# A fused three-stage kernel: block 0's convolution sum moved to TensorE, three weight splits moved behind block 0's first steps

## The reference

```python
# 1. softmax over 7 taps, then a causal 7-tap sum per head (x: 2 x 4096 x 192, 8 heads)
w = weight_gen - np.max(weight_gen, axis=-1, keepdims=True)
w = np.exp(w)
w = w / (np.sum(w, axis=-1, keepdims=True) + 1e-09)
out = np.einsum('bshk,bskhg->bshg', w, x_unf)        # x_unf: rows s-6 .. s of x
# 2. first dense stage, 192 -> 2048 -> 192, with a rational activation
h = x @ w_in
P = a[0] + a[1] * h + a[2] * h2 + a[3] * h3
Q = 1.0 + np.abs(b[0]) * np.abs(h) + np.abs(b[1]) * h2
y = (P / (Q + 1e-6)) @ w_out
# 3. second dense stage, 192 -> 1536 -> 192, RMS norm and a gated activation
xn = x / rms * rms_g
g = xn @ w_gate
silu = g * (1.0 / (1.0 + np.exp(-g)))
return (silu * (xn @ w_val)) @ w_out2
```

## Time and profile before

| | us |
|---|---|
| median of 3 runs | 1444.98 |
| profiled execution | 1445.34 |
| its span, first to last instruction | 1443.5 |
| PE busy | 1368.5 (95%) |
| DVE busy | 1247.1 (86%) |
| ACT busy | 1071.0 (74%) |
| POOL busy | 458.4 (32%) |

### The profile page before, as it was taken

The page is one execution under the profiler, slowest core; times in us unless marked ns, Lnnn a source line. Parts: engine busy times, 40 slices in busy tenths (PEclk is TensorE's granted clock), DMA queues, the critical chain, the costliest instruction groups (busy, mean ns, idle before and its releaser), DMA issues.

```text
span 1443.5 us, 20421 instructions
## 1 busy us (share of the span) xinstructions
PE 1368.5 (95%) x7040; PEld 1221.0 (85%) x7040; DVE 1247.1 (86%) x1524; ACT 1071.0 (74%) x1387; POOL 458.4 (32%) x283
## 2 busy tenths in 40 slices
PE   2676999999999999999999999999999999999999
PEld 2465898888898888889898888989888898998988
DVE  6999998989889898988989899898989989888621
ACT  4676877878787787888778788877878787777521
POOL 2935240434324143432414343241434314200000
PEclk9788999999999999999999999999999999999999
DMA  8200001000000100000010000001000000000000
GB/s 232 82 0 31 1 2 41 1 32 11 30 11 0 41 0 30 11 30 11 0 41 0 30 11 30 11 0 41 0 30 11 30 12 0 12 0 1 12 12 11
DMA packets 12514, 32.30 MB, mean 22 GB/s; under 512 B 1604, under 2 KB 7234, under 8 KB 12480
## 3 DMA queue, kind: packets, MB, share of 16 engines
q1 hardware_dynamic: 11744, 31.61, 6.8%
q10 hardware_dynamic: 736, 0.23, 0.1%
HBM read 25.55 MB, written 6.29 MB: 22 GB/s over the span
## 4 chain that ended last, share of the span: by engine, by line
PE 76%; DVE 11%; ACT 7%; issue 4%; DMA 2%; SPq 0%; ACTq 0%; POOL 0%; DVEq 0%; POOLq 0%
PE dn L681 32%; PE bank L672 9%; PE bank L673 8%; PE bank L674 8%; PE bank L675 8%; PE bank L676 8%; DVE den L607 4%; ACT seed L484 2%; PE bank L688 2%; DVE num L599 2%; DVE num L596 1%; DVE num L612 1%; DVE num L618 1%; ACT L484 1%; DMA glu<-in_moe_w_val_dram 1%
## 5 line engine op out<-in xcount | busy, mean ns | idle before, releaser
L681 PE MATMUL dn<-dn_w,num 128*128 128x192 f32 x2048 | 378.8, 329 | 17.1 <-DVE num L618 9.9
L681 PEld LDWEIGHTS dn<-dn_w,num 128*128 128x128 f32 x2048 | 343.5, 192 | 24.3 <-DVE num L618 8.6
L469 ACT ACTIVATE den<-bank,coef 128x512 f32<-128x512 f32 x256 | 175.5, 686 | 175.8 <-PE bank L676 164.6
L681 PE MATMUL dn<-dn_w,glu 128*128 128x192 f32 x1536 | 280.8, 327 | 5.3 <-DVE glu L643 5.3
L681 PEld LDWEIGHTS dn<-dn_w,glu 128*128 128x128 f32 x1536 | 254.3, 190 | 12.9 <-DVE glu L643 8.9
L596 DVE TENSOR_TENSOR num<-num,bank 128x512 f32<-128x512 f32 x256 | 173.9, 679 | 70.1 <-ACT num L471 68.1
L612 DVE SCALAR_TENSOR_TENSOR num<-num,coef,seed 128x1024 f32<-128x1024 f32 x128 | 183.5, 1435 | 40.8 <-ACT seed L490 40.3
L471 ACT ACTIVATE num<-bank,coef 128x512 f32<-128x512 f32 x256 | 199.5, 779 | 0.0
L618 DVE SCALAR_TENSOR_TENSOR num<-den,num 128x1024 f32<-128x1024 f32 x128 | 193.1, 1510 | 0.0
L597 DVE SCALAR_TENSOR_TENSOR den<-den,coef,bank 128x512 f32<-128x512 f32 x256 | 188.9, 738 | 0.0
L599 DVE SCALAR_TENSOR_TENSOR num<-num,coef,bank 128x512 f32<-128x512 f32 x256 | 188.9, 738 | 0.0
(11 more groups left out here) (86 smaller groups left out, 1983.4 us busy)
## 6 DMA issues: line engine op xcount, KB each, us to landing
x_in<-in_x_dram SPq DMA_DIRECT2D x14, 960.0 KB
out_dram<-y_out SPq DMA_DIRECT2D x16, 384.0 KB, 2.3
w_blk<-in_weight_gen_dram SPq DMA_DIRECT2D x14, 112.0 KB, 2.0
dn_w<-in_moe_w_out_dram SPq DMA_DIRECT2D x1, 1536.0 KB, 20.7
dn_w<-in_moe_w_out_dram SPq DMA_DIRECT2D x1, 1152.0 KB, 10.6
num<-in_moe_w_in_dram SPq DMA_DIRECT2D x1, 768.0 KB, 6.6
num<-in_moe_w_in_dram SPq DMA_DIRECT2D x2, 384.0 KB, 8.2
seed<-in_moe_w_gate_dram SPq DMA_DIRECT2D x1, 768.0 KB, 10.0
```

Of the source, the lines that this page charges most:

```text
L681: done = pe.matmul(banks[:, j // 2, j % 2 * D:(j % 2 + 1) * D], acts[:, j * P:(j + 1) * P], w, start=first and j % 2 == 0, stop=last, skip ...
```

## The change

Six things are done.

1. VectorE makes block 0's seven products into separate buffers (`FIRST`) and adds only two pairs of them (products 3 and 4, and 5 and 6): nine instructions in place of fourteen.
2. TensorE flips each of the five remaining tiles with a matmul against the identity and adds them up in PSUM (`flip_and_add`): 12 matmuls a tile (four with 128 output rows into bank 1, eight with 64 into bank 2), 60 in all, in place of eight transposes.
3. Ahead of them TensorE runs 20 products of the identity with itself.
4. ScalarE splits pieces 5, 6 and 7 in iteration 1 of its order, among block 0's `linear`, `abs` and `root` steps.
5. GpSimd keeps only the low half of piece 4 in the opening; those of 5, 6 and 7 follow block 1's convolution.
6. SP's load of block 1's rows and GpSimd's clearing of the halo wait for the seventh product, not for the sum.

```diff
@@ -21,6 +21,7 @@
 EPS_Q = 1.0 + 1e-6
 EPS_RMS = 1e-6
 GLU_RING = 4
+WARM = 20
 
 
 def program(text):
...
@@ -42,9 +43,9 @@
...
-linear 0 1, root 3 2, square 6 2, silu 4 3, linear 1 1, piece 6 0, square 7 2, linear 2 1, linear 3 1,
-piece 7 0, abs 0 1, linear 4 1, silu 5 3, linear 5 1, abs 1 1, root 0 1, square 0 1, square 1 1, linear 6 1,
+silu 6 3, abs 2 1, linear 7 1, piece 5 1, ss 0 2, silu 7 3, abs 3 1, piece 6 1, silu 8 3, root 1 1, piece 7 1, linear 8 1, linear 9 1,
...
@@ -59,7 +60,7 @@
 """)
 
 POOL_PROGRAM = program("""
-add 6 1, less 0 0, norm 0 0, mul 0 0, mul 1 0, mul 2 0, add 1 0, mul 3 0, add 2 0, mul 4 0, rms 0 2, add 3 0,
+add 6 1, piece 5 2, piece 6 2, piece 7 2, less 0 0, norm 0 0, mul 0 0, mul 1 0, mul 2 0, add 1 0, mul 3 0, add 2 0, mul 4 0, rms 0 2, add 3 0,
 mul 5 0, add 4 0, mul 6 0, add 5 0,
 """)
 
...
@@ -287,6 +287,13 @@
         def slots(rows):
             return rows.rearrange("p (j d) -> p j d", j=SLOTS)
 
+
+        FIRST = [slots(prod[:, 0, :]), slots(prod[:, 1, :]), square[:, :, :], y_out[:, :, :], conv_rows,
+                 xn_t[:, :, 0:D], conv_rows]
+
+        def by_slot(rows):
+            return rows.rearrange("p j (h g) -> p j h g", h=H)
+
         def slot_heads(rows):
             return rows.rearrange("p (j h) g -> p j h g", h=H)
 
@@ -340,7 +347,7 @@
                 load_piece(n)
             src, dst = DOWN[0]
             sp.dma_start(dst[:, :, :], src).then_inc(down_in[0], 16)
-            sp.wait_ge(conv0_ready, 1)
+            sp.wait_ge(tap0, K)
             load_first(1)
             sp.dma_start(w_blk[:, :], w_rows[:, 2 * SLOTS * HK:3 * SLOTS * HK]).then_inc(wgen_in, 16)
             src, dst = DOWN[1]
...
@@ -388,11 +395,10 @@
             def normalised_taps(blk, _):
                 normalise(pool, blk)
 
-            pool.wait_ge(conv0_ready, 1)
+            pool.wait_ge(tap0, K)
             pool.memset(x_in[:, 0:(HALO - SLOTS) * D], 0.0).then_inc(halo0, 1)
             pool.wait_ge(wlo0, BY_DVE)
-            for n in range(BY_DVE, len(PIECES)):
-                piece_low(0, n)
+            piece_low(0, BY_DVE)
 
 
             def tap_product(blk, k):
...
@@ -459,7 +466,6 @@
                 piece_high(0, n)
             x_high(0, 0)
             x_high(0, 1)
-            piece_high(0, 5)
             act.wait_ge(coefs, 2)
 
             def linear(blk, c):
@@ -550,22 +556,17 @@
             normalise(dve, 0)
             dve.wait_ge(sm_norm, 1)
 
-            def first_taps(k):
+            def first_product(k):
                 if k == 0:
                     dve.wait_ge(x_in_ready, x_count(0))
-                    dve.tensor_tensor(conv_heads, slot_heads(rows_of(0)), slot_heads(taps_of(0, 0)), ALU.mult).then_inc(tap0, 1)
-                    return
-                if k > 1:
-                    dve.wait_ge(sum0, k - 1)
-                dve.tensor_tensor(by_head(prod[:, 0, :]), rows_of(k), taps_of(k, 0), ALU.mult).then_inc(tap0, 1)
-                dve.wait_ge(tap0, k + 1)
-                product = slots(prod[:, 0, :])
-                if k < K - 1:
-                    dve.tensor_tensor(conv_rows, conv_rows, product, ALU.add).then_inc(sum0, 1)
-                else:
-                    dve.tensor_tensor(conv_twice, conv[:, :, DA:D], product[:, :, DA:D], ALU.add).then_inc(sum0, 1)
-                    dve.wait_ge(sum0, K - 1)
-                    dve.tensor_tensor(conv_rows, conv_rows, product, ALU.add).then_inc(conv0_ready, 1)
+                elif k == 6:
+                    dve.wait_ge(sum0, 1)
+                dve.tensor_tensor(by_slot(FIRST[k]), slot_heads(rows_of(k)), slot_heads(taps_of(k, 0)), ALU.mult)\
+                    .then_inc(tap0, 1)
+
+            def first_sum(k):
+                dve.wait_ge(tap0, k + 2)
+                dve.tensor_tensor(FIRST[k], FIRST[k], FIRST[k + 1], ALU.add).then_inc(sum0, 1)
 
             def x_low(blk, part):
                 wait(dve, xt_hi, blk * 2 + (part + 1))
@@ -575,8 +576,12 @@
                     dve.tensor_tensor(x_b[DB:P, :], bank[XPOSE_BANK[1]][DB:P, :], x_b[DB:P, :], ALU.subtract)\
                        .then_inc(x_ready, 1)
 
-            for k in range(K):
-                first_taps(k)
+            for k in range(5):
+                first_product(k)
+            first_sum(3)
+            for k in range(5, K):
+                first_product(k)
+            first_sum(5)
             for n in range(2):
                 piece_low(n)
             dve.wait_ge(small_in, 16 * 5)
@@ -689,10 +694,7 @@
                 return done
 
             def transposes(blk, part):
-                if isinstance(blk, int) and blk == 0:
-                    pe.wait_ge(conv0_ready, 1)
-                else:
-                    wait(pe, conv_ready, blk)
+                wait(pe, conv_ready, blk)
                 bank_read(blk, "xpose", part)
                 flip(bank[XPOSE_BANK[part]], conv, part).then_inc(xt_ready, 1)
 
@@ -747,9 +749,30 @@
                 wait(pe, glu_ready, blk * 12 + (m + 1))
                 second_layer(dn2, glu[:, m % GLU_RING, :], dn2_w[:, m, :], m == 0, m == N2 - 1).then_inc(dn2_done, 1)
 
+            def flip_and_add(tile, first, last):
+
+                for j in range(SLOTS):
+                    done = pe.matmul(bank[XPOSE_BANK[0]][:, j * P:(j + 1) * P], tile[:, j, 0:DA], ident[:, :],
+                                     start=first and j == 0, stop=last, skip_group_check=True)
+                if last:
+                    done.then_inc(xt_ready, 1)
+                for j in range(SLOTS):
+                    for half in range(0, P, DB):
+                        done = pe.matmul(bank[XPOSE_BANK[1]][half:half + DB, j * P:(j + 1) * P], tile[:, j, DA:D], ident[:, :],
+                                         start=first and j == 0, stop=last, skip_group_check=True)
+                if last:
+                    done.then_inc(xt_ready, 1)
+
             pe.wait_ge(consts, 3)
-            transposes(0, 0)
-            transposes(0, 1)
+            for n in range(WARM):
+                pe.matmul(bank[XPOSE_BANK[0]][:, 0:P], ident[:, :], ident[:, :], start=True, stop=True)
+            for k in (0, 1, 2):
+                pe.wait_ge(tap0, k + 1)
+                flip_and_add(FIRST[k], k == 0, False)
+            pe.wait_ge(sum0, 1)
+            flip_and_add(FIRST[3], False, False)
+            pe.wait_ge(sum0, 2)
+            flip_and_add(FIRST[5], False, True)
             pe.wait_ge(wlo0, 2)
 
             run_iterations(pe, PE_PROGRAM, {
```

More of the change, by code:

```diff
@@ L44 @@
 square 4 2, x_high 1 1, square 5 2, abs 6 2, silu 0 3, silu 1 3, abs 7 2, silu 2 3, silu 3 3, exp 0 0,
-linear 0 1, root 3 2, square 6 2, silu 4 3, linear 1 1, piece 6 0, square 7 2, linear 2 1, linear 3 1,
-piece 7 0, abs 0 1, linear 4 1, silu 5 3, linear 5 1, abs 1 1, root 0 1, square 0 1, square 1 1, linear 6 1,
-silu 6 3, abs 2 1, linear 7 1, ss 0 2, silu 7 3, abs 3 1, silu 8 3, root 1 1, linear 8 1, linear 9 1,
+linear 0 1, root 3 2, square 6 2, silu 4 3, linear 1 1, square 7 2, linear 2 1, linear 3 1,
+abs 0 1, linear 4 1, silu 5 3, linear 5 1, abs 1 1, root 0 1, square 0 1, square 1 1, linear 6 1,
+silu 6 3, abs 2 1, linear 7 1, piece 5 1, ss 0 2, silu 7 3, abs 3 1, piece 6 1, silu 8 3, root 1 1, piece 7 1, linear 8 1, linear 9 1,
 linear 10 1, square 2 1, silu 9 3, abs 4 1, silu 10 3, linear 11 1, silu 11 3, square 3 1, xn_high 0 2,
@@ L215, in build @@
         sum0 = sem("sum0")
-        conv0_ready = sem("conv0_ready")
         tap_ready = sem("tap_ready")
@@ L430, in _ @@
             run_iterations(pool, POOL_PROGRAM, {"mul": tap_product, "add": tap_add, "rms": rms_inverse,
-                                                "less": peak_taken_off, "norm": normalised_taps}, LAST)
+                                                "less": peak_taken_off, "norm": normalised_taps,
+                                                "piece": piece_low}, LAST)
         @block.scalar
```

## The result

The changed kernel takes **1448.74 us** (1447.17 to 1452.04), the kernel before 1444.74 us (1443.11 to 1447.46), medians of 14 runs each. The ratio is 1.0029, with a 95% interval of 1.0022 to 1.0036: 4.0 us slower, and the interval leaves out an equal time. That lies just inside what the prediction calls no change (0.3%), on its slow side, as forecast; forecast were 1447.8 us and +2.8. The profiled execution lasted 1448.36 us (span 1446.6) against 1445.34 (span 1443.5), 3.0 us more.

What follows compares the result with a forecast made beforehand. VectorE was taken to bound the first 150 us, TensorE from 160 us on. An opening gain of 5.3 us against 8.1 us of new waiting gave +2.8 on 1444.98, so 1447.8 us, range 1442.0 to 1451.0.

Steps and rivals of the forecast that it cites:

- The convolution is worth nothing: Opening: 4.3 us off VectorE's convolution turn nearly all into idle time, as `x_high` waits for piece 4; 0.1 us gained.
- TensorE's flips cost nothing: Opening, block 0: 60 flip products are done by 19.5 us, or 24.5 at the lower clock; cost 0, ends 0 and 0.3.
- the rival that gave TensorE too little time: Opening: an fp32 product costs twice a transpose, `horner` 0 at 41.5, about +10.5 us, 1455.5; chance 0.03.
- `horner` 0 at 29.2: Opening, VectorE's first `horner`: starts at about 29.2 us in place of 34.67, 5.5 us earlier.
- Block 1's rows at 39.0: Start of GpSimd's block 1 convolution: its rows land at 39.0 us, with ends of 37.0 and 41.0.
- the main case: Whole kernel: halves block whole, rows land between 38 and 40.5; +1.8 to +4.3 us, 1446.8 to 1449.3; chance 0.52.
- rows at 40.4: Variant of the step-by-step working to the last `py`: block 1's rows landing at 40.4 us give +4.1.
- Three halves block three or four steps, 8.1 us: Behind block 1's convolution, 67 to 83 us: VectorE's `qy`, `newton` and `py` wait for GpSimd's low halves, 8.1 us.
- the rival that a half blocks less than its length: Cheaper collision beside GpSimd's halves, or rows before 38: -1.5 to +1.5 us, 1445.0; chance 0.18.
- the one that it does not collide: GpSimd's halves do not block VectorE: the whole 5.3 us gain stays, 1439.7 us; chance 0.13.
- VectorE has no idle time in which to give it back: After the last `py` near 83 us: the 2.8 us loss stays, and TensorE from 150 us on waits for it.
- in all of every window: Steady part from 160 us: TensorE busy 40.00 of 40.00, a fixed sum that the change does not touch.

Runs made afterwards that it cites:

- e4: The changed kernel's opening alone (flips, identity products, earlier rows), with the splits of pieces 5 to 7 where they were before: 1446.02 us, 1.0005 to the kernel before.
- e6: The changed kernel without the 20 identity products: 1447.33 us, 1.0021 to the kernel before.
- e5: The kernel before with only the splits of pieces 5 to 7 moved on ScalarE and GpSimd: 1448.12 us, 1.0022 to the kernel before.
- e1: The changed kernel with GpSimd clearing the low-half tiles of pieces 5 to 7 instead of subtracting: 1441.98 us, 0.9983 to the kernel before.
- e3: The changed kernel with GpSimd's low-half subtractions cut into 256 columns each: 1442.27 us, 0.9981 to the kernel before.
- e7: The changed kernel with piece 5 split in the opening again on both engines: 1445.35 us, 1.0006 to the kernel before.
- e8: The changed kernel with piece 5 split in the opening and GpSimd's halves cut into 256 columns: 1443.43 us, 0.9987 to the kernel before.
- e10: e9 plus 18 identity products behind the last flip and piece 2's low half ahead of `x_low`: 1431.05 us, 0.9908 to the kernel before.
- e12: e9 with GpSimd's convolution instructions cut in four, one slot each, instead of two: 1432.80 us, 0.9918 to the kernel before.
- e9: e8 with GpSimd's convolution products and additions of blocks 1 to 15 cut in two (one addition excepted): 1431.22 us, 0.9901 to the kernel before.
- e2: The changed kernel with GpSimd's low-half subtractions cut into 512 columns each: 1445.39 us, 0.9998 to the kernel before.
- e11: The kernel before with only GpSimd's convolution instructions of blocks 1 to 15 cut in two: 1434.16 us, 0.9924 to the kernel before.

## Why the prediction came out as it did

The mechanism was right. One term of the sum was mis-sized: when block 1's rows land. It moved the result by about 1.1 us.

- *The convolution is worth nothing.* VectorE was idle 5.94 us behind it, and e4 shows no change. Right.
- *TensorE's flips cost nothing.* Right, but the prices were wrong, and that it did no harm was in part luck. A full fp32 product takes 0.27 us at the higher level for my 0.11. I had misread: the profile has two records for each fp32 product (the 20 identity products show as x40, and the 1024 products of the first stage's `down1` as x2048), so its 24 records of 4.06 us are 12 products of 0.34 us, not 24 of 0.17. Scaled to 128 columns that is 0.23. The premise of the rival that gave TensorE too little time, a product that costs twice a transpose, was thus about true: in e6, at the slower pace, a full one takes 0.49 us for the transposes' 0.24. It did no harm because 40 of the 60 products go into 64 rows and cost half (0.13, or 0.24 at the slower pace), and because all ran at the higher level; even at e6's mixed pace they were done at 23.11. A tile takes 2.1 us instead of 1.4, and the last is still done 3.3 us early. The 20 identity products took 7.00 us for my 4.8 at most and ended 0.85 before the first flip.
- *`horner` 0 at 29.2.* It came at 30.52. Of the 1.3 us, 0.8 is piece 4, whose data landed later in this execution (22.97 for 22.17); it holds `x_high`, and so `up1`, which starts at 26.56 for my 25.8. The other 0.5 is the five matmuls and the `linear` behind them, 2.57 and 1.39 us for my 2.2 and 1.27.
- *Block 1's rows at 39.0.* They came at 40.51, at the edge of the 38 to 40.5 of the main case. **This is the term that was mis-sized**: the prediction's own line for rows at 40.4 reads +4.1, and `horner` 12 came 3.9 us later. GpSimd's convolution took 28.3 us from there, as forecast, ended at 68.77 for my 67.3, and the `py` beside it ended 1.1 after that, so by this working an earlier `horner` 0 alone would have met the same end. (No run has that alone. In e6 `horner` 0 was 1.4 earlier and the rows 0.6, but the convolution took 29.2 us, and `horner` 12 came at 83.31, 0.9 earlier: its length is not as fixed as I took it.) SP's issue of the rows, begun at 17.21, lasted 15.39 us, until 32.60, and the rows were there 7.9 us after that. In e5, which begins at 22.30, it ended at 30.89 and the rows came 7.6 later. In e1, e3, e6, e7, e8, e10 and e12, begun at 16.2 to 17.3, it ended at 32.0 to 32.5 and they came 7.5 to 7.8 later, at 39.7 to 40.2; in e9 it ended at 32.7 and they came at 40.70, in e2 at 35.6 and 43.88. So the landing follows the end of the issue by nearly 8 us, which would have made about my 39.0 of the 31.53 of before; the end is what moved, later by 1.1 us. The prediction had said that the earlier start would not change it. The three runs that start at 22.0 to 22.4 (before, e5, e11) end at 30.8 to 31.5, the eleven that start at 16.2 to 17.3 at 31.6 (e4) to 35.6. That speaks for the earlier start, but the wait was not changed alone, so it stays open.
- *Three halves block three or four steps, 8.1 us.* Measured were 8.0. That each step ends 1.1 us after its half held to 0.1 us. e1 and e3 show by removal that this waiting, and its length, are the loss; e5 that it needs nothing of the convolution; the rival that a half blocks less than its length, and the one that it does not collide, fell. The rule of the Trainium skill (SBUF — State Buffer, Who interferes with whom) is that the shared port pair is an exclusive lock, that whoever comes second is blocked for the whole instruction of the first, and that a VectorE instruction with two SBUF inputs meets it where GpSimd reads SBUF. This trace agrees at 1536 columns: 4.43 us is 3.3 of waiting and 1.1 of its own. What the page says besides, that a GpSimd instruction which only writes does not contend, agrees with e1's 1.21.
- *VectorE has no idle time in which to give it back.* Not quite: at 84 us the changed kernel is 3.9 us late, when `xn_t` starts for block 0 only 3.0 (214.60 for 211.64), and the profiled execution ends 3.0 later. Between the two stand VectorE's waits for ScalarE's `seed`, two in either kernel; after and before:

```profile
177.59 2.61 DVE L617 SCALAR_TENSOR_TENSOR num<-num,coef,seed 128x1024 f32<-128x1024 f32 x1 [0.26 <-ACT seed L496]
199.36 1.28 DVE L617 SCALAR_TENSOR_TENSOR num<-num,coef,seed 128x1024 f32<-128x1024 f32 x1 [0.38 <-ACT seed L496]
```

```profile
174.99 1.48 DVE L612 SCALAR_TENSOR_TENSOR num<-num,coef,seed 128x1024 f32<-128x1024 f32 x1 [1.40 <-ACT seed L490]
196.40 1.28 DVE L612 SCALAR_TENSOR_TENSOR num<-num,coef,seed 128x1024 f32<-128x1024 f32 x1 [1.16 <-ACT seed L490]
```

They shrink by 1.9 us, and the `num` at 177.59 takes 1.1 longer beside GpSimd: 0.8 of the 0.9. This was read, not tried. The medians of the runs differ by 4.0, the profiled executions by 3.0; the interval of the runs' difference, 3.2 to 5.2 us, does not hold 3.0, so what other executions lose beyond this one is open. The traces show that the giving back is not in every execution: from `horner` 12 to `xn_t` of block 0 it is 131.4 us in the kernel before, in e1, e3 and e6, and 130.4 in the changed kernel, e5 and e7. That the 3.0 of the profiled executions lies so near the forecast 2.8 is luck: the rows cost 1.1 more and 0.9 came back.

- *What I did not see.* I read TensorE as full from 160 us on and left the steady part alone. The window that I showed, 160 to 200 us, is full (40.00 of 40.00), but "in all of every window" was false: 400 to 900 us has 497.29 of 500. Twelve waits of half a microsecond lie there and around it, and e9 and e11 remove 5.3 us of them, more than the 4.0 that the change lost.

## What to carry to other kernels

In this kernel, where GpSimd and VectorE steps with two inputs in SBUF lay beside each other, the step that came second waited for what was left of the other's instruction: before moving such work, look at what VectorE step it will lie beside, and try it in shorter instructions (here 256 columns instead of 1536, two slots instead of four). Cutting has an end: each more instruction cost GpSimd 0.14 us, and four parts were no better than two. And what shorter work on one engine is worth is known only with the queue behind it: ScalarE's pieces held back all that VectorE and TensorE had finished early (e4).

## What was unexpected of the hardware

- Clearing 1536 columns on GpSimd (1.35 us) beside a VectorE step with two SBUF inputs costs that step nothing (1.21); subtracting as many costs it 3.3 us.
- An fp32 product of 128 columns takes 0.27 us at the higher clock level and 0.13 into 64 rows, while transposes of 128 columns took 0.24 at the lower level. Such a product has two records in the profile, a transpose one.
- TensorE's granted clock was at the lower level again after 5.52 us without work (0.50 from 27 to 31 us, matmuls of 512 columns 0.43 apart from 27.12 us), and at the higher one in e10, after 2.05 us without work behind its 18 identity products (1.00 from 26.5 to 30 us). In e6, whose work on TensorE began only at 10.00 us, the first `up1` came after 2.29 us without work, with its matmuls 0.43 apart; whether the somewhat longer pause or the shorter work ahead of it made the difference, the two do not tell. The granted clock of the profile has to be read with the distances: in the kernel before it reads 1.00 from 27 to 31 us, with the first matmuls 0.43 apart as well. The rows of e10:

```profile
26.75 0.47 PE L691 MATMUL bank<-x_ah,up_ah 128*128 128x512 f32 x1 [2.05 <-DVE x_b L590]
...
27.29 0.40 PE L693 MATMUL bank<-x_ah,up_al 128*128 128x512 f32 x1
```

- SP's issue of block 1's rows lasted 8.6 to 19.0 us behind the loads issued ahead of it, and where GpSimd waited for these rows they were there 7.5 to 8.3 us after the issue ended, whenever it had begun. What ends such an issue no run shows.
